# Two feed-forward layers behind an attention on one core: another form of the second layer's quotient, its out product in three f32r passes, one PSUM operand per VectorE operation

## The reference

```python
h = x @ w_in1                                  # layer 1
x = (max(h, 0) + alpha * min(h, 0)) @ w_out1
h = x @ w_in2                                  # layer 2
P = a0 + a1*h + a2*h**2 + a3*h**3
Q = 1 + |b0|*|h| + |b1|*h**2
out = (P / (Q + 1e-6)) @ w_out2
```

## Time and profile before

| | us |
|---|---|
| median of 3 runs (lowest, highest) | 1774.72 (1773.73, 1775.84) |
| span of the profiled execution | 1772.3 |
| DVE busy | 1608.6 (91%) |
| PE busy | 1659.1 (94%) |
| ACT busy | 1478.1 (83%) |
| POOL busy | 1013.8 (57%) |
| from the first to the last Q (L515, 384 of them) | 402.0 to 1759.1 |

### The profile page before, as it was taken

The page is one execution under the profiler, slowest core; times in us unless marked ns, Lnnn a source line. Parts: engine busy times, 40 slices in busy tenths (PEclk is TensorE's granted clock), DMA queues, the critical chain, the costliest instruction groups (busy, mean ns, idle before and its releaser), DMA issues.

```text
span 1772.3 us, 25002 instructions
## 1 busy us (share of the span) xinstructions
PE 1659.1 (94%) x5615; PEld 929.9 (52%) x5615; DVE 1608.6 (91%) x2365; ACT 1478.1 (83%) x2707; POOL 1013.8 (57%) x968
## 2 busy tenths in 40 slices
PE   2899999999999999999999999999999999999965
PEld 2677777754555455555554555554555455555531
DVE  5676767618999999999999999999999999999998
ACT  2455555549999999999999999999999999999986
POOL 0111111106777777777777777777777777777775
PEclk8999999999999999999999999999999999999999
DMA  7100000000000000000000000000000000000000
GB/s 227 48 18 24 18 24 18 6 1 1 7 7 0 6 6 6 6 0 6 6 6 0 6 6 6 6 0 6 6 6 0 6 6 6 6 0 6 6 7 6
DMA packets 12200, 23.42 MB, mean 13 GB/s; under 512 B 1536, under 2 KB 1680, under 8 KB 11920
## 3 DMA queue, kind: packets, MB, share of 16 engines
q1 hardware_dynamic: 10896, 19.93, 3.6%
q10 hardware_dynamic: 1280, 3.22, 0.6%
HBM read 16.85 MB, written 6.29 MB: 13 GB/s over the span
## 4 chain that ended last, share of the span: by engine, by line
DVE 60%; PE 16%; issue 15%; ACT 5%; DVEq 0%; ACTq 0%; POOLq 0%
DVE area L532 16%; DVE banks L515 14%; DVE area L529 13%; DVE area L540 12%; PE banks L638 7%; DVE area L535 3%; PE banks L629 2%; PE banks L550 2%; PE banks L552 2%; PE banks L551 2%; ACT area L327 1%; DVE x_lo L523 1%; PE banks L703 1%; DVE area L519 1%; ACT area L399 1%
## 5 line engine op out<-in xcount | busy, mean ns | idle before, releaser
L268 POOL TENSOR_TENSOR area<-area 128x512 f32<-128x512 f32 x384 | 495.3, 1290 | 393.4 <-DVE area L532 365.1
L550 PE MATMUL banks<-x_hi,win_lo 128*128 (+1 forms) x768 | 481.9, 627 | 53.2 <-DVE area L540 27.8
L261 POOL TENSOR_TENSOR area<-area 128x512 f32<-128x512 f32 x384 | 489.2, 1274 | 43.4 <-ACT area L390 43.4
L532 DVE SCALAR_TENSOR_TENSOR area<-area,neg_a 128x512 f32<-128x512 f32 x384 | 492.6, 1283 | 0.0
L737 PE MATMUL banks<-area,wout 128*128 128x512 f32 x768 | 416.0, 623 | 6.6 <-POOL area L268 4.4
L703 PE MATMUL banks<-neg_part,wout 128*128 128x512 f32 x768 | 392.4, 593 | 0.5 <-ACT neg_part L404 0.5
L552 PE MATMUL banks<-x_hi,win_hi 128*128 (+1 forms) x768 | 303.6, 395 | 0.0
L551 PE MATMUL banks<-x_lo,win_hi 128*128 (+1 forms) x768 | 302.4, 394 | 0.0
L550 PEld LDWEIGHTS banks<-x_hi,win_lo 128*128 128x128 f32 x768 | 144.5, 188 | 284.3 <-DVE area L540 178.9
L515 DVE SCALAR_TENSOR_TENSOR banks<-area,abs_b,banks 128x512 f32<-128x512 f32 x384 | 284.4, 741 | 4.7 <-ACT area L389 4.7
L540 DVE SCALAR_TENSOR_TENSOR area<-banks,neg_a,area 128x512 f32<-128x512 f32 x384 | 283.7, 739 | 1.1 <-POOL area L261 1.1
(11 more groups left out here) (75 smaller groups left out, 1528.7 us busy)
## 6 DMA issues: line engine op xcount, KB each, us to landing
area<-in_kv_dram SPq DMA_DIRECT2D x24, 256.0 KB, 5.6
area<-in_q_dram SPq DMA_DIRECT2D x24, 256.0 KB, 2.6
out_dram<-area SPq DMA_DIRECT2D x24, 256.0 KB, 2.0
area<-in_moe_w_in_dram ACTq DMA_DIRECT2D x2, 1024.0 KB, 11.5
neg_part<-in_w_sr_dram ACTq DMA_DIRECT2D x1, 64.0 KB, 12.0
al_rows<-in_moe_alpha_dram ACTq DMA_DIRECT2D x1, 8.0 KB, 5.4
ab_raw<-in_moe_a_dram ACTq DMA_DIRECT2D x1, 2.0 KB, 7.7
ab_raw<-in_moe_b_dram ACTq DMA_DIRECT2D x1, 1.0 KB, 8.9
```

Source lines behind the costliest of these rows:

```text
L261: nc.gpsimd.tensor_tensor(cubic[:, b, :], sq[:, b, :], lin_p[:, b, :], ALU.mult).then_inc(s["cubic_done"], 1)
L268: nc.gpsimd.tensor_tensor(rational[:, 1 - b, :], residue[:, 1 - b, :], ratio[:, 1 - b, :], ALU.mult).then_inc(s["rat_done"], 1)
L532: nc.vector.scalar_tensor_tensor(ratio[:, 1 - b, :], poly[:, 1 - b, :], neg_a[:, 0:1], rcp[:, 1 - b, :], ALU.add, ALU.mult).then_inc(s["ra ...
L550: nc.tensor.matmul(dst, w[1], x[0], start=start, stop=False)
```

## The change

The quotient is computed in another way, the second out product takes the split form, and the pipeline is laid out anew:

- g_hi = (h-part of P + a0) x rcp, rounded to f32r; product = Q x g_hi; residue = P - product; g_lo = residue x rcp, rounded to f32r. The second out product multiplies wout2_hi, wout2_lo with g_hi, g_lo in three f32r matmuls. P is now written back over h in its PSUM bank, so H2 has three banks; H1, the bank of layer 1's hidden product, has one instead of two.
- DVE's five operations each read one operand from PSUM and one from SBUF. POOL keeps two products of SBUF tiles.
- Layer 2 trails by 19 slots (hidden product, middle part), 20 (reciprocal, g_hi, residue), 21 (g_lo) and 22 (out product). In a PE slot the hidden product of layer 2 comes first.
- The loop's body holds three groups (48 slots) and runs 7 times; three groups are unrolled ahead as before.
- wout2 is loaded into an area shared with x_hi, and split by ACT (high part) and DVE (low part) in attention step 1. neg_a and its operation are gone.

```diff
-LAG2 = 18
+IN2, MID, BACK, LOW, OUT2 = 19, 19, 20, 21, 22
+TRIPLE = 3
-        H1, ACC1, QV, H2, ACC2 = (0, 1), 2, (3, 4), (5, 6), 7
+        H1, ACC1, QV, H2, ACC2 = 0, 2, (3, 4), (5, 6, 1), 7
 # layer_steps
-            with eng.Fori(3, GROUPS) as it:
-                for i in range(BLOCKS):
-                    slot(it, i)
+            with eng.Fori(1, GROUPS // TRIPLE) as triple:
+                for g in range(TRIPLE):
+                    for i in range(BLOCKS):
+                        slot(triple * TRIPLE + g, i, g * BLOCKS + i)
 # attention, ACT and DVE, only in step k == 1
+                    act.wait_ge(s["ld_out2"], 16)
+                    nc.scalar.activation(wout2_hi[:], raw_out2, ACT.Copy).then_inc(s["out2_hi_done"], 1)
+                    dve.wait_ge(s["out2_hi_done"], 1)
+                    nc.vector.tensor_tensor(wout2_lo[:], raw_out2, wout2_hi[:].bitcast(F32), ALU.subtract)...
 # POOL layers: cubic of block s-19 as before, then of block m = s-21
+                    pool.wait_ge(s["resid_done"], m + 1)
+                    after(pool, s["m2_done"], m - 1)
+                    nc.gpsimd.tensor_tensor(g_lo[:, b, :], residue[:, b, :], rcp[:, b, :], ALU.mult)
 # ACT layers, new order: Relu(s-1); Square(s-19); Ln(s-20); [x_hi at i == 1]; Identity(s-19);
 #   Exp(s-20), after glo_done m-1; Abs(s-19), after prod_done m-1; [y_t at i == 5]
 # DVE layers, new order, BACK: m = s-20, MID: m = s-19
+                    dve.wait_ge(s["rcp_done"], m + 1)
+                    dve.wait_ge(s["poly_done"], m + 1)
+                    after(dve, s["m2_done"], m - 1)
+                    nc.vector.scalar_tensor_tensor(g_hi[:, b, :], banks[:, H2[h], :], ab_raw[:, 0:1], rcp[:, b, :],
+                                                   ALU.add, ALU.mult)                       # BACK
                     ... Q into banks[QV], after absb_done                                      # MID
+                    nc.vector.scalar_tensor_tensor(product[:, b, :], banks[:, QV[b], :], C_Q, g_hi[:, b, :].bitcast(F32),
+                                                   ALU.add, ALU.mult)                       # BACK
                     ... [y_out at i == 5, waits for y2_t_ready]
+                    nc.vector.scalar_tensor_tensor(banks[:, H2[h], :], banks[:, H2[h], :], ab_raw[:, 1:2], cubic[:, b, :],
+                                                   ALU.mult, ALU.add)                       # MID
                     ... [x_lo at i == 0, waits for y1_hi_done]
+                    nc.vector.scalar_tensor_tensor(residue[:, b, :], banks[:, H2[h], :], ab_raw[:, 0:1], product[:, b, :],
+                                                   ALU.add, ALU.subtract)                   # BACK
 # PE layers, new order
+                    after(pe, s["resid_done"], m - 2)
+                    hidden(H2[h], win2_hi, win2_lo, c, g).then_inc(s["h2_ready"], 1)          # m = s-19
                     ... [linear product], out product of layer 1 for block s-2; [transposes at i == 6]
+                    after(pe, s["neg_done"], n)
+                    hidden(H1, win1_hi, win1_lo, i, it).then_inc(s["h1_ready"], 1)            # n = s
+                    pe.wait_ge(s["glo_done"], m + 1)
+                    split_product(banks[:, ACC2, :], (wout2_hi.., wout2_lo..), (g_hi.., g_lo..), ...)   # m = s-22
```

More of the change, by code:

```diff
@@ L108, in build @@
         w_in1_t = cut(BLOCKS, P)
+        raw_out2 = cut(ff)
+        pooled_t = cut(keys)
+        q_in = early[:, 2 * tokens - 2 * GROUP:2 * tokens].rearrange("p (b c) -> p b c", b=2)
         w_sr_sb = neg_part[:, 0, 2 * P:3 * P]
         pooled = neg_part[:, 0, 0:2 * P].rearrange("p (b c) -> p b c", b=2)
-        pooled_t = wout2.rearrange("p b c -> p (b c)")[:, 0:keys]
-        used[0] = 0
+        area = sb("area", [P, 32 * 256])
+        cut = cutter(area, 32 * 256)
         probs = cut(2, TILES, keys)
         expd = cut(2, keys)
[L117 to L124, removed]
+        probs_t = neg_part
+        cut = cutter(area, 32 * 256)
+        sq, lin_p, cubic, log_q, rcp, product, residue = (cut(2, GROUP) for _ in range(7))
+        y_t, y_out = cut(GROUP), cut(GROUP)
+        g_hi, g_lo = q_hi, q_lo
         banks = ctx.enter_context(nc.psum_tensor("banks", [P, 8, GROUP], F32))
@@ L262, in layers @@
                                             ALU.mult).then_inc(s["cubic_done"], 1)
[L263 to L269, removed]
+                if live(it, i, LOW, N1):
+                    m, b = it * BLOCKS + (i - LOW), (phase - LOW) % 2
+                    pool.wait_ge(s["resid_done"], m + 1)
+                    after(pool, s["m2_done"], m - 1)
+                    nc.gpsimd.tensor_tensor(g_lo[:, b, :], residue[:, b, :], rcp[:, b, :],
+                                            ALU.mult).then_inc(s["glo_done"], 1)
             layer_steps(pool, layers)
@@ new lines, in _, with layers @@
+            act.reg_load(scale_a3, ab_raw[0:1, 3:4].bitcast(mybir.dt.int32))
+            def layers(it, i, phase):
+                if live(it, i, 1, N1):
+                    n, b = it * BLOCKS + (i - 1), (i - 1) % 2
+                    act.wait_ge(s["h1_ready"], n + 1)
+                    after(act, s["m1_done"], n - 1)
+                    nc.scalar.activation(neg_part[:, b, :], banks[:, H1, :], ACT.Relu,
+                                         scale=-1.0).then_inc(s["neg_done"], 1)
+                if live(it, i, MID, N1):
+                    m, b, h = it * BLOCKS + (i - MID), (phase - MID) % 2, (phase - MID) % 3
+                    act.wait_ge(s["h2_ready"], m + 1)
@@ L387, in layers @@
                     after(act, s["q_done"], m - 1)
                     after(act, s["cubic_done"], m - 1)
-                    nc.scalar.activation(sq[:, b, :], banks[:, H2[b], :], ACT.Square).then_inc(s["sq_done"], 1)
-                    nc.scalar.activation(lin_p[:, b, :], banks[:, H2[b], :], ACT.Identity, bias=neg_a[:, 2:3],
-                                         scale=scale_a3).then_inc(s["linp_done"], 1)
-                if i == 0 and group_live(it, 1):
+                    nc.scalar.activation(sq[:, b, :], banks[:, H2[h], :], ACT.Square).then_inc(s["sq_done"], 1)
@@ L393, in layers @@
+                if live(it, i, BACK, N1):
+                    m, b = it * BLOCKS + (i - BACK), (phase - BACK) % 2
+                    act.wait_ge(s["q_done"], m + 1)
+                    nc.scalar.activation(log_q[:, b, :], banks[:, QV[b], :], ACT.Ln, bias=C_Q * 2.0 ** -LN_SHIFT,
+                                         scale=2.0 ** -LN_SHIFT).then_inc(s["ln_done"], 1)
+                if i == 1 and group_live(it, 1):
                     act.wait_ge(s["m1_done"], it * BLOCKS)
@@ L701, in layer_1_out @@
                         split_product(banks[:, ACC1, :], (lin_hi[:], lin_lo[:]), (x_hi[:, cols], x_lo[:, cols]), True, False)
[L702 to L703 removed]
+                    pe.wait_ge(s["neg_done"], n + 1)
+                    nc.tensor.matmul(banks[:, ACC1, :], wout1[:, c, :], neg_part[:, b, :], start=False,
                                      stop=(c == BLOCKS - 1)).then_inc(s["m1_done"], 1)
[L706 to L713 removed]
+                if i == 6 and group_live(it, 2):
```

203 lines of the change are left out of this document (92 added, 111 removed).

## The result

The changed kernel takes 1784.28 us (median of 4, 1782.87 to 1785.55) against 1774.22 (median of 4, 1772.02 to 1775.84) for the kernel before beside it: ratio 1.0054, 95% interval 1.0042 to 1.0066. It is slower by half a per cent, where I forecast 1764. Its profiled span is 1783.1 us, 10.8 more than before.

What follows compares the result with a forecast made beforehand. DVE was taken to bound the kernel, L532 sitting out most of POOL's product. Against the 1772.3 us span, -29 + 4 - 2 + 2.5 + 14 = -10.5 gave 1761.8; with 2.4 for the median, 1764, range 1747 to 1779.

Steps and rivals of the forecast that it cites:

- first slots: Slots with layer 1 alone: with one H1 bank each hidden product waits for the Relu before, 1.67 us each, +4.
- weights' split: Attention step 1: ACT copies wout2's high part, DVE subtracts; between 0 and 4.2 us, taken as +2.5, once.
- the end: From the last Q's start to the end: about 11 us instead of 13.2, -2.
- loop's end: Jumps of the 48-slot body: engines wait for their first instructions, 2.3 us at each of 6 jumps, +14.
- loop one: Layer slots: residue, PE's matmuls through the out product, g_hi, residue; 6.62 us for two slots, 3.31 per slot.
- the term of -29: Layer slots, first to last Q: group of 55.5 us instead of 56.75 over 383 slots, -30 taken as -29.
- hop back 0.04, taken like the other: Layer slots: from the out product's end on PE to g_hi's start on DVE, 0.04 us.
- counts twice over: Rival, layer slots: further hops make the loops bind harder, 3.38 us per slot; 1789 with fetches, 1775 without; chance 0.13.
- DVE's part: Layer slots: five operations of 0.66, 0.66, 0.60, 0.66, 0.66, 3.24 us per slot, none held up by POOL.
- group's extras: Once-per-group work (x_lo, linear product, y_out, transposes) falls on the slots' chain: 2.5 us per group.
- wait ahead of y_out: Slot 5 of each group: DVE waits for PE's transposes ahead of the output copy, 0.7 us.
- bound of 56.9: Group time in us if each new wait costs some 0.08 us more, which is all of the gain.

Runs made afterwards that it cites:

- three: Changed kernel with a third buffer for g_hi and g_lo, so g_hi waits for the out product before last: 1754.35 us, ratio 0.9884.
- outf32: Changed kernel with layer 2's out product as one f32 matmul of wout1 and g_hi instead of three f32r, g_lo left out: 1813.37 us, ratio 1.0218.
- waits: Changed kernel with g_hi's three waits reordered, the one for the out product first instead of last: 1782.34 us, ratio 1.0037.
- before48: Kernel before with only the layer loop's body changed, three groups (48 slots) per body instead of 16 slots: 1785.43 us, ratio 1.0056.
- hint: Changed kernel with the layer loop's closing branch announced at the top of the body on every engine: 1772.67 us, ratio 0.9986.
- yout: Changed kernel with the output's copy y_out moved behind P in slot 5 on DVE: 1784.86 us, ratio 1.0061.
- keep: Kernel before, arithmetic and f32 out products kept, with P in PSUM, three H2 banks, one H1, 48-slot body, announced jump: 1640.47 us, ratio 0.9250.

## Why the prediction was wrong

The forecast span was 1761.8, the measured one 1783.1. The 21.3 us by the steps:

| step | forecast | measured | difference |
|---|---|---|---|
| slots, first to last Q, without jumps | -29 | 1359.9 - 13.5 - 1357.1 = -10.7 | +18.3 |
| ahead of them: first slots | +4 | (409.6 - 402.0) - 4.0 = +3.6 | -0.4 |
| attention and weights' split | +2.5 | +4.0 | +1.5 |
| the end | -2 | +0.4 | +2.4 |
| loop's end, 6 jumps | +14 | +13.5 | -0.5 |

- **The step that failed is the sum of loop one, the term of -29.** The mechanism was right: the loop, its two waits and every duration in it stand in the trace, and three and outf32 show that it binds. Its price was 6.62 us and is 6.72, of which 0.09 is one number, "hop back 0.04, taken like the other", measured at 0.13. With 383/2 turns, 0.10 us is 19 us. Every other part came out within 0.01: to PE 0.06, the matmuls 3.20, g_hi to the residue's end 3.33. I had the warning among the rivals ("counts twice over", 3.38 per slot, 1789 with the fetches; it became 3.36 and 1784), with a chance of 0.13. The change's own gain was so small against its bound that a hop copied from an operation whose waits are built otherwise decided the sign, together with the jumps. The experiment waits shows that the hop follows from the order of the waits: 0.06 us and 6.66 for two slots. That the whole kernel gains by it is not shown.
- **The loop's end was right** in place and count; that its sum of 14 met 13.5 is partly luck. I had 2.3 us per jump. before48 and hint show it from both sides: 1.7 us per jump alone, which is 10 in all; in two jumps the clock's fall, which I had not counted, adds another 1.7. That the pause is the loading of instructions is the nearest reading of the packets and of hint; no row shows which engine waited for which packet. It took both to make the kernel slower: 1784 less the 18 of the failed step is 1766, and without the jumps' cost, in hint, 1772.67 was measured.
- **DVE's part** was right: 0.66, 0.66, 0.60, 0.66 and 0.66, no operation held up by POOL. So was g_lo at 1.28 us.
- **The group's extras**, 2.5 us, were 56.33 - 16 x 3.36 = 2.57. The wait ahead of y_out was 0.45 instead of 0.7, and yout, which takes it away, gained 0.15 us per group. The bound of 56.9 that I gave for 0.08 us more in each new wait comes to 56.7 by my own terms (3.39 per slot).
- **The first slots** took 1.65 us each once the attention was done (forecast 1.67).
- **The end.** I shortened it by 2 us; it is 0.4 longer. Its matmuls, which I priced at full speed, run at the lower level of the granted clock: the last out product takes 1.64 us instead of the 0.9 that I took, and the transposes 1.11 instead of 0.66. The kernel before had a low clock there too, for less of the time. Windows from the last Q to the end, in the changed kernel and then in the kernel before:

```profile
1769.50:1783.10 13.60, 6.06 (x13) 3.21 (x13) 5.56 (x9) 1.82 (x3) 3.90 (x4) 0.55 0.06 20
```
```profile
1759.10:1772.30 13.20, 6.24 (x10) 1.72 (x10) 5.96 (x10) 1.95 (x4) 4.62 (x4) 0.68 0.05 20
```
- **The weights' split.** The attention's last x_lo starts at 375.17 us instead of 371.17. DVE's subtraction is as long as priced, and DVE waited for ACT's copy before it. PE then waited for DVE in its turn, and its next matmuls ran at a lower clock:

```profile
75.04 2.29 DVE L514 TENSOR_TENSOR wout_lo<-early,wout_hi 128x2048 fp32r<-128x2048 f32 x1 [2.45 <-ACT wout_hi L355]
...
77.99 2.08 PE L661 MATMUL banks<-neg_part,values 128*128 128x512 f32 x2 [3.91 <-DVE neg_part L483]
```

The granted clock of the changed kernel was 0.72 in 78:84 (and in 60:66), where the kernel before has 1.00. In the seven other kernels that have this split that x_lo starts at 374.8 to 378.0 us, in the four without it, the kernel before among them, at 371.2 to 372.1. So the term is 3 to 7 us from one execution to the next, and the changed kernel's profile was at its low end.

What I did not see at all is keep. I priced what L532 lost (0.6 us per slot), but not what the rest of the change gave up for it: the split out product saves PE 0.17 us that the changed kernel does not need by itself, while the new quotient costs DVE 3.24 us instead of 2.91 per slot and puts DVE and PE into one loop through g_hi's buffer. P in PSUM brings 7.5% with the banks, PE's new wait and the body that it was run with.

## What to carry to other kernels

When no engine is full, follow each loop of waits around and price every hop in it from an operation whose waits are built in the same way; with a hundred turns or more a tenth of a microsecond can decide the sign. A third buffer is the cheap cure (30 us here); the late semaphore as the first of several waits shortened each group by 0.48 us, though not the total. Each cure must be followed to the loop that stands next. And before the arithmetic is rewritten to cure one slow operation, move that operation's operand by itself: here this, with the banks it needs, took 133 us off, where the whole rewrite added 10.

## What the runs showed of the hardware that was not expected

- An operation behind two separate waits that carries the third itself started 0.13 us after the modelled end of the matmul; with the late semaphore first in order it was 0.06 (waits).
- At some jumps the granted clock fell to the level of 1.2 GHz for a few us when PE had paused: in two of six jumps of the changed kernel and of outf32, one of six in three, three in yout, all six in waits. A jump then cost 3.0 to 3.6 us instead of 1.6 to 2.0. PE's pauses there lasted 1.6 to 2.2 us, with and without a fall, so their length does not tell them apart. In before48, where PE paused for at most 1.2 us, the clock fell at none.
- Announcing the jump took its cost away, though the queues still load instructions (31 packets instead of 68 in 600:1600).
- POOL's product costs the same with f32r output, 1.28 us on the mean of 384 against 1.29 with f32 output in the same kernel.
